# Spreads of the value means issued by ScalarE, and each pair-batch's values ahead of the next keys on the load queue

## The reference

```python
block, window = (32, 16)
nb = S // block
scale = 1.0 / np.sqrt(D)
k_sum = k.reshape(B, H, nb, block, D).max(axis=3)
v_sum = v.reshape(B, H, nb, block, D).mean(axis=3)
...
scores_s = scores_s + np.log(block)
scores_l_m = np.where(mask_l, scores_l, -1000000000.0)
scores_all = np.concatenate([scores_l_m, scores_s], axis=-1)
...
a = a / (np.sum(a, axis=-1, keepdims=True) + 1e-09)
v_all = np.concatenate([v, v_sum], axis=2)
return np.matmul(a, v_all).astype(np.float32)
```

## Time and profile before

| | us |
|---|---|
| median of 3 timed runs | 622.24 |
| lowest, highest | 619.99, 626.68 |
| the profiled execution's own time | 619.3 |
| its span, first to last instruction | 617.2 |
| PE busy in the span | 581.2 (94%) |
| DVE busy | 443.0 (72%) |
| ACT busy | 261.6 (42%) |
| POOL busy | 147.2 (24%) |

### The profile page before, as it was taken

The page is one execution under the profiler, slowest core; times in us unless marked ns, Lnnn a source line. Parts: engine busy times, 40 slices in busy tenths (PEclk is TensorE's granted clock), DMA queues, the critical chain, the costliest instruction groups (busy, mean ns, idle before and its releaser), DMA issues.

```text
span 617.2 us, 9768 instructions
## 1 busy us (share of the span) xinstructions
PE 581.2 (94%) x3360; PEld 473.0 (77%) x3360; DVE 443.0 (72%) x839; ACT 261.6 (42%) x556; POOL 147.2 (24%) x158
## 2 busy tenths in 40 slices
PE   4587899999999999999999989999999999999995
PEld 3465678888888888888888867788888888888884
DVE  5467798765343333356765699999999999999996
ACT  4477731110131110311110855566766566766564
POOL 6255640000030000120000566622222222222220
PEclk9999999999999999999999999999999999999999
DMA  8477544000000000023322200000100000100001
GB/s 252 100 212 246 191 163 184 0 1 0 1 1 0 0 0 0 0 68 103 103 102 102 69 1 0 1 0 1 68 0 0 0 0 0 69 1 0 1 1 68
DMA packets 13535, 32.55 MB, mean 53 GB/s; under 512 B 1728, under 2 KB 4416, under 8 KB 13504
## 3 DMA queue, kind: packets, MB, share of 16 engines
q1 hardware_dynamic: 13360, 31.99, 16.1%
q10 hardware_dynamic: 144, 0.13, 0.1%
HBM read 27.79 MB, written 3.15 MB: 50 GB/s over the span
## 4 chain that ended last, share of the span: by engine, by line
PE 46%; DVE 35%; issue 9%; ACT 3%; DMA 3%; SPq 2%; DVEq 1%; POOL 0%; POOLq 0%
PE bank L533 22%; PE bank L585 21%; DVE ratio L981 9%; DVE numer L963 6%; DVE ratio L975 5%; DVE numer L961 5%; DVE ratio L970 5%; DVE hhi L988 4%; DMA kraw<-kT 3%; ACT prob L665 2%; SPq L262 1%; PE bank L502 1%; PE bank L519 1%; DVE hlo L992 1%; PE bank L483 1%
## 5 line engine op out<-in xcount | busy, mean ns | idle before, releaser
L533 PE MATMUL bank<-xhi,whi 128*128 (+1 forms) x384 | 149.8, 390 | 0.1
L533 PE MATMUL bank<-xhi,wlo 128*128 (+1 forms) x384 | 149.4, 389 | 0.0
L533 PE MATMUL bank<-xlo,whi 128*128 (+1 forms) x384 | 149.4, 389 | 0.0
L443 POOL TENSOR_TENSOR denom<-denom,habs 128x512 f32<-128x512 f32 (+1 forms) x49 | 62.3, 1273 | 251.0 <-ACT denom L736 251.0
L678 ACT ACTIVATE hsq<-bank 128x512 f32<-128x512 f32 x48 | 28.8, 600 | 213.2 <-PE bank L533 213.1
L533 PEld LDWEIGHTS bank<-xhi,whi 128*128 128x128 f32 x384 | 72.1, 188 | 15.2 <-issue 0.3
L533 PEld LDWEIGHTS bank<-xhi,wlo 128*128 128x128 f32 x384 | 72.1, 188 | 15.1
L533 PEld LDWEIGHTS bank<-xlo,whi 128*128 128x128 f32 x384 | 72.1, 188 | 14.7
L600 PE MATMUL bank<-whi,hhi 128*128 128x512 f32 x192 | 75.9, 395 | 7.6 <-DVE hlo L992 7.6
L600 PE MATMUL bank<-wlo,hhi 128*128 128x512 f32 x192 | 74.8, 390 | 0.0
L600 PE MATMUL bank<-whi,hlo 128*128 128x512 f32 x192 | 74.8, 390 | 0.0
(11 more groups left out here) (69 smaller groups left out, 862.2 us busy)
## 6 DMA issues: line engine op xcount, KB each, us to landing
wraw<-w SPq DMA_DIRECT2D x32, 512.0 KB, 4.1
vwin<-vw SPq DMA_DIRECT2D x16, 288.0 KB, 5.4
q<-qT SPq DMA_DIRECT2D x8, 384.0 KB, 6.0
out<-osb SPq DMA_DIRECT2D x12, 256.0 KB, 2.1
kraw<-kT SPq DMA_DIRECT2D x7, 384.0 KB, 6.1
vwin<-vsum SPq DMA_DIRECT2D x32, 36.0 KB
kraw<-kT SPq DMA_DIRECT2D x2, 128.0 KB, 2.4
kraw<-kT ACTq DMA_DIRECT2D x1, 128.0 KB, 2.7
```

The costliest lines, as they stand in the source:

```text
L443: g.tensor_tensor(denom[:, i, cols], denom[:, i, cols], habs[:, i, cols], ALU.mult).then_inc(q_done, 1)
L533: last = mm(hps[j % 2][:, :], W[a][:, j, kt * P:(kt + 1) * P], X[b][:, kt, bass.ds(CH * c, CH)], start=kt == 0 and i == 0, stop=kt == KT - ...
```

## The change

`spread_summary` leaves SP and is called by ScalarE inside `exps`, one strip behind one exponential: for pairs 0, 1 and 2 all four strips in one group, for pairs 3 to 7 two strips in each of two groups, the first being the group behind SUMMARY_AT[n]. There it waits for `vsum_copied`, and from pair 4 on also for the last output of pair n-4. The summary of pair 2 moves from group 3 to group 4. SP's loads are written in one loop: queries n, values n, keys n+1, then the first weights. Lines of the new kernel: exponentials L638, spreads L653, summary copy L661, copy to `probT` L684; on SP queries L249, values L255, keys L240, first weights L258, later weights L263.

```diff
-SUMMARY_AT = [0, 1, 3] + [GPB * n - 4 for n in range(3, NB)]
+SUMMARY_AT = [0, 1, 4] + [GPB * n - 4 for n in range(3, NB)]
...
-        load_q(1)
-        load_k(2)
-        load_vwin(1)
-        load_q(2)
-        for n in range(NB):
-            if n == 0:
-                load_vwin(2)
-            elif n + RING < NB:
-                load_vwin(n + RING)
-            if n + RING < NB:
-                load_k(n + RING)
-            if n == 0:
-                spread_summary(0)
-                load_vwin(RING)
-                spread_summary(1)
-            if n + RING < NB:
-                load_q(n + RING)
...
-            if n == 1:
-                spread_summary(2)
-            if 0 < n and n + 2 < NB:
-                spread_summary(n + 2)
+        for n in range(1, NB):
+            load_q(n)
+            load_vwin(n)
+            if n + 1 < NB:
+                load_k(n + 1)
+            if RING <= n < RING + EARLY:
+                load_first(n - RING)
+        sp.dma_start(ca[:, :], coef_a.partition_broadcast(P)).then_inc(coef_in, 16)
+        sp.dma_start(braw[:, :], coef_b.partition_broadcast(P)).then_inc(coef_in, 16)
+        for j in range(EARLY, FT // 2):
+            load_weights(w1, j, *landing(j))
...
-        def exps(G, r):
+        def exps(G, r, spreads=()):
 
             act.wait_ge(s_free, done(2, G))
             for u in range(GU):
                 last = a.activation(prob[r][:, u, :], prob[r][:, u, :], ACT.Exp, bias=lowest[r][:, u:u + 1],
                                     scale=-1.0, accum_out=rowsum[r][:, u:u + 1])
-            last.then_inc(exp_done, 1)
+                if u < len(spreads):
+                    if u == GU - 1:
+                        last.then_inc(exp_done, 1)
+                    spread_summary(*spreads[u])
+            if len(spreads) < GU:
+                last.then_inc(exp_done, 1)
+
+        def spread_summary(n, t):
+
+            act.wait_ge(vsum_copied, n + 1)
+            if n >= V_RING:
+                act.wait_ge(o_done, done(2, GPB * (n - V_RING + 1) - 1))
+            rows = KW + 2 * GPB * t
+            act.dma_start(vwin[n % V_RING][rows:rows + 2 * GPB, :, :],
+                          vsum[n % 2][32 * t:32 * t + 2 * GPB, :].unsqueeze(1).to_broadcast([2 * GPB, NW, P])
+                          ).then_inc(vsum_in[n % V_RING], 16)
...
-        exps(2, 2)
+        exps(2, 2, [(0, t) for t in range(4)])
         for G in range(GROUPS):
+            spreads = []
+            for n in range(1, NB):
+                first = SUMMARY_AT[n] + 1
+                if n < RING and G == first:
+                    spreads = [(n, t) for t in range(4)]
+                elif n >= RING and G == first:
+                    spreads = [(n, 0), (n, 1)]
+                elif n >= RING and G == first + 1:
+                    spreads = [(n, 2), (n, 3)]
...
-                exps(G + 3, (G + 3) % P_RING)
+                exps(G + 3, (G + 3) % P_RING, spreads)
```

More of the change, by code:

```diff
@@ L255, in load_vwin @@
                 sp.dma_start(vwin[n % V_RING][0:KW, half, :], vw[n][:, half, :]).then_inc(vw_in[n % V_RING], 16)
[L257 to L264, removed]
         def load_first(j):
```

## The result

The changed kernel is slower: 643.52 us median of 4 runs (641.21 to 645.23) against 622.68 us median of 4 runs of the kernel before, ratio 1.0327 with a 95% interval of 1.0258 to 1.0395. The profiled execution took 645.23 us, its span is 643.1 (before: 617.2). The forecast was 615.4 with a range of 611 to 629.

A forecast was written before the change was run, and what follows sets the result against it. TensorE is busy in 94% of the span, so the end of attention, slowed by waits for keys behind SP's spreads, passes one for one into the kernel's end; -1.0 - 5.0 + 0.3 = -5.7 us gave 615.4, range 611 to 629.

The forecast's parts named there:

- Part 1: Key loads on SP no longer behind spreads: VectorE's 8.4 us wait for keys goes; ScalarE's 6.6 us per pair comes next.
- Part 2: 32 spread issues move to ScalarE, 0.77 us each on its sequencer, mostly hidden: 0.3 us per pair, in all 6.95.
- the sum: Whole kernel: -1.0 to output 6, -5.0 over outputs 6 to 18, +0.3 for groups 19 and 20: -5.7 us.
- half hidden: Rival, chance 0.22: ScalarE's sequencer is not ahead, +0.45 us per issue, 8.2 per pair; +1.5 us, 622.6.
- Part 3: Start, spread of pair 0: output 0 at 19.4 instead of 22.04 us, -2.6, between bounds of -5.1 and 0.
- Part 4: Outputs 3 and 6: output 3 keeps -2.6; the later summary gives back 1.6, so output 6 comes 1.0 us earlier.
- late landing: Rival, chance 0.16: spreads share full DMA engines and gain nothing at the start; +2.6 on the forecast, -3.1 us, 618.0.
- not hidden: Rival, slower side, chance 0.16: each DMA issue waits until ScalarE drains and costs 0.77 us, 9.4 per pair; +9.4, 630.5.

The follow-up runs named there:

- the fastest kernel: The changed kernel with the spreads back on SP and the summary of pair 2 back in group 3: 616.32 us, ratio to before 0.9904.

## Why the prediction was wrong

The sign was wrong and the time outside the range. The step that failed is the landing of a spread, in parts 3 and 4.

- *Part 1, keys no longer behind spreads: right that the wait goes, too low a pace.* The row of VectorE waiting for keys is gone. What is left was put at 6.65 us per pair without issues; with the spreads on SP it is 6.96. The changed kernel itself never showed the gain: outputs 6 to 14 took 21.42 us, 0.7 less than before.
- *Part 2, issues on ScalarE: right for two issues in a group.* 0.3 us per pair forecast, 0.25 measured with issues alone. Over the whole kernel they came to 2.9 us instead of 1.5 (4 x 0.3 + 0.3), most of it in the first pairs, to which the sum gave nothing. For the groups with four issues the rival "half hidden" describes the rows (0.85 us per exponential), for those with two the forecast does.
- *Part 3, the start: wrong.* The bounds were -5.1 and 0 us, with 0 for a spread that is as late as behind all loads on SP. Neither holds. The -5.1 had the spread run as if alone, right behind its issues; its first packet went at 18.1 us, as before. And 0 was no bound: beside loads on another queue the spread's packets took some 9.5 us instead of 3.1, and output 0 came 6.2 us later. The step looked at the DMA share (1.02) and read it as a queue to wait in; it never counted packets, though the spread's size (36 KB an issue in pieces of one row of 512 B) was in the code.
- *Part 4, outputs 3 and 6: wrong for the same reason.* 3.08 us from issue to landing was read from a moment in which the engines had room (DMA share 0.41 from 28 to 32 us). In the changed kernel SP no longer waits for spreads, so its loads go out when outputs are done, which is when ScalarE issues. Landings took 6.95 us and more at the outputs that waited. The summary of pair 2 in group 4 was priced at less than 2 us; beside loads it cost some 6. Against the sum, output 6 came 18.4 us later than before instead of 1.0 earlier, and outputs 6 to 18 took 5.8 us more instead of 5.0 less.
- *The rival "late landing": the right place at a tenth of its price.* It was given 0.16 and +2.6 us, at output 0 alone, for engines that are shared and full. The landings of four spreads were late, and most of the 24.8 us by which output 23 came later lies there. No rival had it as the slower side; "not hidden", which did, did not happen.
- *The sentence of the Trainium skill* that a second issuer saves only issue time ("DMA: Bandwidth & Descriptors", section "Issuing engines are not separate DMA queues") pointed at the right place. These runs show more than it says: the second queue was not neutral, it cost.

Beside the 20.8 us the runs give: holding loads back beside the same issues -16.6, spreads on SP instead of ScalarE -25.5 (643.52 to 618.06), the summary of pair 2 -6.2 (part of the same landings), ScalarE's issues by themselves about 3. These overlap and don't add up.

## What to carry to other kernels

Here a transfer of many small packets did not become faster on a queue of its own while another queue had large packets in flight: it started no earlier and took three times as long. In the common queue it waited only for what was ahead of it, and its place there could be chosen. Before moving a transfer that someone waits for, count its packets and theirs, and ask what the mover's old queue will do in the time it no longer waits: here the waits on SP had also kept the loads away from the spreads. A landing time read from a quiet moment is no price for a busy one.

## What the runs showed of the hardware that was not expected

The share of a queue beside a busy one went up with its own packet size (0.06 to 0.09 MB in 4 us for 512 B and 1 KB) and with a shorter packet on the other (0.08 MB), each less than in proportion. And a queue with work got nothing for a while: pair 0's spread, issued from 12.46 us on, moved its first packet at 18.1.

A long wait costs more than itself. TensorE's granted clock in three stretches of the changed kernel, the second with the wait before output 3:

```profile
28.00:36.00 8.00, 7.63 (x132) 5.92 (x132) 3.16 (x20) 4.18 (x17) 0.99 (x1) 1.00 0.16 56
36.00:44.00 8.00, 0.79 (x20) 0.64 (x14) 2.47 (x14) 2.59 (x11) 3.25 (x4) 0.67 0.72 203
44.00:52.00 8.00, 8.00 (x134) 6.04 (x131) 4.07 (x22) 4.21 (x17) 1.42 (x2) 0.69 0.18 56
```

It was all but idle from 36 to 43 us (0.79 us busy in 8) and its clock fell from 1.00 to a mean of 0.67, that is to the lower level of 1.2 GHz for part of the stretch. Behind it 16 output products took 1.12 us instead of 0.69, and output 4 came 4.5 us behind output 3 instead of 2.6; part of that is the clock, part the refilling of the chain of engines, and the two were not separated.

In the fastest kernel TensorE has a gap of 0.96 us in the middle of the 16 products of output 13 (14 and then 2 of them), again with no releaser:

```profile
56.82 0.68 PE L509 MATMUL bank<-probT,vwin 120*64 120x64 f32 x14
58.46 0.33 PE L509 MATMUL bank<-probT,vwin 120*64 120x64 f32 x2 [0.96 <-issue]
```

The kernel before with the keys early has two such gaps (0.52 and 1.65 us), the output products of the other kernels have none. Their cause was not tried.
